# Attention probabilities kept 160 columns wide and turned in four row quarters

## The reference

```
B, H, S, D = 2, 8, 768, 64            # n_global 8, n_local 96
scores = q @ k.T / sqrt(D) + bias     # bias: -slope[h] * distance
keep = (pos_k < n_global) | ((rel >= 0) & (rel < n_local))
a = softmax(where(keep, scores, -1e9))
x = a @ v                             # (B, S, H * D) = (2, 768, 512)
h = relu(x @ w_in)                    # d_ff = 1024
x2 = (h * sigmoid(conv3(h))) @ w_out
g = relu(x2 @ w_in2);  u, v = halves of g
out = (u * (w_spatial @ layernorm(v) + b_spatial)) @ w_out2
```

## Time and profile before

| what | value |
|---|---|
| median of 3 runs (lowest, highest) | 361.33 us (361.33, 361.51) |
| the profiled execution | 361.26 us, span of its instructions 359.5 us |
| PE busy | 351.6 us, 2891 matmuls |
| DVE, ACT, POOL busy | 215.7, 177.7, 89.2 us |
| granted clock of PE, mean | 1.000 |

### The profile page before, as it was taken

How to read it: one execution, slowest core, us unless ns; L and a number is a source line. 1 busy time by engine, 2 the same in 40 slices (tenths; PEclk the granted TensorE clock), 3 DMA queues, 4 the chain that set the end, 5 groups by cost and what they waited for, 6 DMA issues and landing times.

```text
span 359.5 us, 7397 instructions
## 1 busy us (share of the span) xinstructions
PE 351.6 (98%) x2891; PEld 321.8 (90%) x2891; DVE 215.7 (60%) x572; ACT 177.7 (49%) x451; POOL 89.2 (25%) x165
## 2 busy tenths in 40 slices
PE   7889999999999999999999999999999999999996
PEld 3558989998899999999889999998999999998885
DVE  6896898778776697789693942115853444441000
ACT  4887668776767688652464622114652111112112
POOL 4899796445554000000120300003400000000000
PEclk9999999999999999999999999999999999999999
DMA  7962342333314033302000000010341000001222
GB/s 215 400 238 67 97 122 83 123 129 113 112 46 162 2 117 119 116 19 100 0 2 1 2 0 0 2 43 2 119 133 45 0 0 2 0 2 60 106 100 94
DMA packets 12233, 27.77 MB, mean 77 GB/s; under 512 B 1568, under 2 KB 4256, under 8 KB 12192
## 3 DMA queue, kind: packets, MB, share of 16 engines
q1 hardware_dynamic: 11904, 27.10, 22.3%
q10 hardware_dynamic: 288, 0.13, 0.2%
HBM read 24.08 MB, written 3.15 MB: 76 GB/s over the span
## 4 chain that ended last, share of the span: by engine, by line
PE 92%; DVE 4%; DMA 1%; issue 1%; POOL 1%; ACT 0%; DVEq 0%
PE bank L1587 20%; PE bank L1589 20%; PE bank L1588 20%; PE bank L1543 19%; PE bank L1522 5%; PE bank L1498 5%; PE bank L1450 3%; DVE p_sb L1072 2%; DMA counts<-in_n_keys 1%; DVE denom L1081 0%; DVE xT L1094 0%; POOL p_sb L635 0%; ACT p_sb L735 0%; DVE table L1051 0%; DVE pt_sb L1089 0%
## 5 line engine op out<-in xcount | busy, mean ns | idle before, releaser
L1543 PE MATMUL bank<-xT,w_hi 128*128 128x384 f32 x256 | 69.5, 344 | 0.0
L635 POOL TENSOR_SCALAR p_sb<-p_sb,denom 128x256 f32<-128x256 f32 (+1 forms) x96 | 47.1, 508 | 38.2 <-DVE denom L1083 38.2
L735 ACT ACTIVATE p_sb<-p_sb,row_min 128x256 f32<-128x256 f32 (+1 forms) x96 | 46.3, 486 | 17.7 <-DVE row_min L1072 17.6
L1543 PEld LDWEIGHTS bank<-xT,w_hi 128*128 128x128 f32 x256 | 45.8, 188 | 0.3 <-issue 0.2
L1543 PE MATMUL bank<-xT,w_lo 128*128 128x384 f32 x128 | 44.0, 344 | 0.0
L1109 DVE SCALAR_TENSOR_TENSOR c_sb<-h_sb,conv_sb,c_sb 128x382 f32<-128x382 f32 (+1 forms) x64 | 42.6, 666 | 2.3
L1587 PE MATMUL bank<-g_hi,w_hi 128*128 128x386 f32 (+1 forms) x128 | 43.3, 338 | 0.0
L1589 PE MATMUL bank<-g_hi,w_lo 128*128 128x386 f32 (+1 forms) x128 | 43.2, 337 | 0.0
L1588 PE MATMUL bank<-g_lo,w_hi 128*128 128x386 f32 (+1 forms) x128 | 43.1, 337 | 0.0
L1072 DVE CUSTOM_DVE_ANT_0 p_sb<-bank,table 128x256 f32<-128x256 f32 (+1 forms) x96 | 33.0, 397 | 8.1 <-PE bank L1450 7.9
L656 POOL TENSOR_SCALAR rstd<-mean_var 128x1 f32<-128x1 f32 x12 | 4.7, 392 | 129.2 <-DVE mean_var L1137 129.2
(11 more groups left out here) (96 smaller groups left out, 784.1 us busy)
## 6 DMA issues: line engine op xcount, KB each, us to landing
stage<-in_weights SPq DMA_DIRECT2D x17, 512.0 KB, 3.3
v_sb<-in_v SPq DMA_DIRECT2D x8, 390.0 KB, 3.9
k_sb<-in_k SPq DMA_DIRECT2D x8, 384.0 KB, 4.2
out_dram<-out_sb SPq DMA_DIRECT2D x11, 256.0 KB, 2.0
q_sb<-in_q SPq DMA_DIRECT2D x13, 192.0 KB, 2.5
v_sb<-in_v SPq DMA_DIRECT2D x6, 260.0 KB, 3.7
k_sb<-in_k SPq DMA_DIRECT2D x5, 256.0 KB, 4.0
stage_late<-in_weights SPq DMA_DIRECT2D x2, 512.0 KB, 11.4
```

The costliest lines, as they stand in the source:

```text
L635: nc.gpsimd.tensor_scalar(probs_h, probs_h, denom[:, u % SLOTS, h:h + 1], 1.0, ALU.mult, ALU.mult).then_inc(scaled, 1)
L735: nc.scalar.activation(p_sb[:, u % SLOTS, h, 0:n], p_sb[:, u % SLOTS, h, 0:n], ACT.Exp, bias=row_min[:, u % SLOTS, h:h + 1], scale=-1.0, a ...
L1543: last = nc.tensor.matmul(h_bank(j)[:, 0:C], w, x, start=r == 0, stop=r == F1_GROUP - 1)
```

## The change

**Layout.** A row of probabilities now holds only the 160 columns that its quarter of 32 rows needs (`NEAR`), with 96 columns of zeros on either side (`PAD`). All four quarters are biased with one table, `near_table`, which ACT copies together at the start from four pieces of the old table. DVE clears the right pads after the table is built, before the first bias; POOL clears the left ones.

**Turning.** A block of 128 keys is turned by four transposes, one for each quarter of 32 rows; each reads 128 columns of its own window in the padded row, and the four write into four banks (`quarters`). Three units lie beside each other in these four banks, and so does the output of attention (`xt_ps`, the last 128 columns of three of them). In triples 0 to 3 PE waits before each turn for the copy of the unit before; in later triples it turns three units in a row, and ACT copies after the third. Weighing starts when all three are copied. Before the next triple is turned, PE waits for `x_copied`.

**Output.** ACT first copies the output of attention raw to SBUF (`copy_x`, `x_raw`); `round_x` and `rest_of_x` then read it there.

**Order.** Scores run three triples ahead from triple 4 on (in triple 4 a second scoring stands in the middle of the first layer's matmuls), the 24 matmuls of the first layer come in one run, and ACT's and DVE's orders follow. The warm-up has 6 matmuls, 32 transposes, and 3 and 3 matmuls.

```diff
-WARM = (8, 3, 3, 3)
+WARM = (6, 8, 3, 3)
+PAD = P - PART
+AT_X = TG * P
-        p_sb = att("p_sb", [P, SLOTS, 2, 2 * P])
+        near_table = att("near_table", [P, NEAR])
+        p_sb = att("p_sb", [P, SLOTS, 2, PAD + NEAR + PAD])
+        x_raw = att("x_raw", [P, 2, C])
+        quarters = psum("quarters", [P, 4, 512])
         def score_cols(u, h):
             p, tt = divmod(u, TG)
-            bank = banks[(2, 5)[h] if tt == 2 else (6, 7)[h] if p == 1 else h]
-            at_col = tt % 2 * 2 * P
-            return bank[:, at_col:at_col + keys(u)]
+            bank = banks[(6 if u == 2 or p in (2, 4) else 0) + h]
+            return bank[:, tt * NEAR:tt * NEAR + near(u)]
-        xt_ps = banks[4]
+        xt_ps = quarters[:, 0:TG, AT_X:AT_X + P]
+        def turned_ps(u):
+            at_col = u % TG * P
+            return quarters[:, :, at_col:at_col + 2 * blocks_of(u) * PART].rearrange("p s (m q) -> p m s q", q=PART)
-        ALONE = TG * (HP + 1)
+        ALONE = TG * (HP + 2)
...
+            nc.gpsimd.memset(p_sb[:, :, :, 0:PAD], 0.0).then_inc(pads, 1)
...
             def copy_pt(u):
-                act.wait_ge(turned, u + 1)
+                act.wait_ge(turned, u + 1 if u < GU else TG * (u // TG + 1))
                 wait_if(act, weighed, u + 1 - PT_SLOTS)
-                n = keys(u)
-                nc.scalar.copy(pt_sb[:, u % PT_SLOTS, :, 0:n], pt_ps(u)[:, :, 0:n]).then_inc(pt_in, 1)
+                nc.scalar.copy(turned_sb(u), turned_ps(u)).then_inc(pt_in, 1)
+            def copy_x(p):
+                wait_if(act, x_lo, p - 1)
+                wait_apart(act, weighed, TG * (p + 1))
+                nc.scalar.activation(x_raw[:, p % 2, :].rearrange("p (t n) -> p t n", t=TG), xt_ps, ACT.Copy
+                                     ).then_inc(x_copied, 1)
             def round_x(p):
-                wait_apart(act, weighed, TG * (p + 1))
-                nc.scalar.activation(xT[:, g % 2, 0, hp, :], xt_ps[:, 0:C], ACT.Copy).then_inc(x_hi, 1)
+                wait_apart(act, x_copied, p + 1)
+                nc.scalar.activation(xT[:, g % 2, 0, hp, :], x_raw[:, p % 2, :], ACT.Copy).then_inc(x_hi, 1)
...
             for u in range(GU):
                 if u < TG and not turned_on_dve(u):
                     copy_pt(u)
                 soften(u + TG)
+                if u % TG == 0 and u > 0:
+                    copy_x(u // TG - 1)
                 if u >= TG and not turned_on_dve(u):
                     copy_pt(u)
                 if u % TG == 0 and u > 0:
                     round_x(u // TG - 1)
             for p in range(HP, ALL_TRIPLES):
                 u = TG * p
+                copy_x(p - 1)
+                round_x(p - 1)
+                if p == HP:
+                    for tt in range(TG):
+                        soften(u + TG + tt)
                 for tt in range(TG):
-                    if p + 1 < ALL_TRIPLES:
-                        soften(u + TG + tt)
-                    if tt == 2:
+                    copy_pt(u + tt)
+                    if tt == 1:
                         relu_h(2 * (p - F1_FIRST))
-                    copy_pt(u + tt)
-                    if tt == 0:
-                        round_x(p - 1)
+                    if p + 2 < ALL_TRIPLES:
+                        soften(u + 2 * TG + tt)
                 relu_h(2 * (p - F1_FIRST) + 1)
+            copy_x(ALL_TRIPLES - 1)
             round_x(ALL_TRIPLES - 1)
...
             build_table()
+            nc.vector.memset(p_sb[:, :, :, PAD + NEAR:], 0.0).then_inc(pads, 1)
...
-            invert_sums(ALONE - 1, 1)
+            for u in range(GU + 2, ALONE):
+                invert_sums(u, 1)
+                if u + 2 < ALONE:
+                    bias_scores(u + 2)
             for p in range(HP, ALL_TRIPLES + 1):
                 u = TG * p
-                for tt in range(TG):
-                    if p + 1 < ALL_TRIPLES:
-                        bias_scores(u + TG + tt)
-                rest_of_x(p - 1)
                 if p == HP:
+                    rest_of_x(p - 1)
                     path_tests()
+                if p + 2 < ALL_TRIPLES:
+                    for tt in range(TG):
+                        bias_scores(u + 2 * TG + tt)
+                if p > HP:
+                    rest_of_x(p - 1)
...
             def turn_probs(u):
-                if u > GU and u % TG:
+                if u == 1:
+                    pe.wait_ge(pads, 2)
+                if 0 < u < GU:
                     wait_pt(pe, u - 1)
+                if u > 0 and u % TG == 0:
+                    pe.wait_ge(x_copied, u // TG)
+                n = blocks_of(u)
                 for h in range(2):
                     pe.wait_ge(scaled, 2 * u + h + 1)
-                    for c in range(0, keys(u), P):
-                        last = nc.tensor.transpose(pt_ps(u)[:, h, c:c + P], p_sb[:, u % SLOTS, h, c:c + P], ident[:])
+                    for k in range(n):
+                        for i in range(4):
+                            rows = slice(i * PART, (i + 1) * PART)
+                            at_key = PAD + k * P - (0 if n == 1 else i * PART)
+                            at_col = u % TG * P + (h * n + k) * PART
+                            last = nc.tensor.transpose(quarters[:, i, at_col:at_col + PART],
+                                                       p_sb[rows, u % SLOTS, h, at_key:at_key + P], ident[rows, rows])
                 last.then_inc(turned, 1)
             def weigh(u):
                 if tt == 0:
-                    wait_if(pe, x_lo, pg)
+                    wait_pt(pe, u)
+                    wait_pt(pe, u + 1)
+                    wait_pt(pe, u + 2)
...
             for p in range(ALL_TRIPLES):
                 for tt in range(TG):
                     turn_probs(TG * p + tt)
-                    if p == 0 and tt == 0:
-                        warm(WARM[3])
-                    if p == 0 and tt == 1:
-                        third_scores(1)
-                    if p >= F1_FIRST:
-                        for _ in range(F1_STEP // TG):
-                            f1(f1_next)
-                            f1_next += 1
-                if p + 2 < ALL_TRIPLES:
-                    scores(p + 2)
+                    if p < HP and tt == 1:
+                        scores(p + 2)
+                if p >= F1_FIRST:
+                    for i in range(F1_STEP):
+                        if p == HP and i == F1_STEP // 2:
+                            scores(p + 2)
+                        f1(f1_next)
+                        f1_next += 1
                 for tt in range(TG):
                     weigh(TG * p + tt)
+                if HP <= p < ALL_TRIPLES - 3:
+                    scores(p + 3)
```

More of the change, by code:

```diff
@@ L298, in build_program @@
         tables = sem("tables")
+        near_in = sem("near_in")
+        pads = sem("pads")
         path_in = sem("path_in")
@@ L314, in build_program @@
         scaled = sem("scaled")
+        x_copied = sem("x_copied")
         x_hi = sem("x_hi")
@@ L409, in place, with near, blocks_of, probs_of @@
             return g, g // 2, hp, tt, TG * (g % 2) + tt
-        def keys(u):
-            return P if place(u)[4] == 0 else 2 * P
+        def near(u):
+            return P if place(u)[4] == 0 else NEAR
+        def blocks_of(u):
+            return 1 if place(u)[4] == 0 else 2
+        def probs_of(u, h):
+            return p_sb[:, u % SLOTS, h, PAD:PAD + near(u)]
+        def turned_ps(u):
+            at_col = u % TG * P
+            return quarters[:, :, at_col:at_col + 2 * blocks_of(u) * PART].rearrange("p s (m q) -> p m s q", q=PART)
+        def turned_sb(u):
+            return pt_sb[:, u % PT_SLOTS, :, 0:blocks_of(u) * P].rearrange("p h (k s q) -> p (h k) s q", q=PART, s=4)
         def turned_on_dve(u):
@@ L810, in _ @@
             nc.scalar.activation(spare[:], minus_half[:], ACT.Exp, bias=minus_half[:], scale=-1.0)
+            act.wait_ge(tables, COUNT_STEPS + 3)
+            for i in range(4):
+                rows, at_col = slice(i * PART, (i + 1) * PART), AT_LATER + i * PART
+                nc.scalar.copy(near_table[rows, :], table[rows, at_col:at_col + NEAR]).then_inc(near_in, 1)
             for u in range(TG):
@@ L1072, in bias_scores @@
                     nc.vector.tensor_tensor_reduce(
-                        out=p_sb[:, u % SLOTS, h, 0:n], in0=score_cols(u, h),
-                        in1=table[:, at_col:at_col + n],
+                        out=probs_of(u, h), in0=score_cols(u, h),
+                        in1=table[:, AT_T0:AT_T0 + P] if t == 0 else near_table[:],
                         scale=slope(2 * hp + h) * UNIT, scalar=FAR, op0=ALU.add, op1=ALU.min,
@@ L1441, in score @@
                 g, _, hp, tt, t = place(u)
-                near = slice(0, P) if t == 0 else slice(part * PART, part * PART + NEAR)
                 at_key = (0, 0, 2 * P)[t] if t < TG else tt * 2 * P
+                first = at_key if t == 0 else at_key + part * PART
```

(23 more changed lines are left out.)

85 lines of the change are left out of this document (33 added, 52 removed).

## The result

The changed kernel takes 378.64 us (median of four runs, 377.62 to 379.78) against 361.33: the ratio is 1.048, 95% interval 1.045 to 1.051, so it is slower by 17.3 us. The forecast was 366.0 with a range of 362.2 to 373.5: the direction was right, the time lies 5 us above the range. The profiled run took 378.83 us, its span is 377.0.

What follows compares the result with a forecast made beforehand. An engine loop paces the kernel up to 28.92 us, PE's own instructions afterwards. Terms 1.7 + 3.7 + 2.4 - 3.7 + 0.4 - 0.5 + 0.3 + 0.3 = +4.6 on 361.3 give 366.0 us, range 362.2 to 373.5.

Steps and rivals of the forecast that it cites:

- If it falls to 1.2 GHz: Triples 1 to 3: if waits drop PE's clock, weighing and turns take about 1.2 us more per triple; chance 0.11.
- D: Rival: PE's longer waits in the loop of triples 1 to 3 lower the granted clock, giving 369.6 us; chance 0.11.
- case E: Rival: only instruction issue limits the quads, 0.027 us each less, -3.3 us, giving 362.7 us; chance 0.06.
- Triples 1 to 3: Shared PSUM banks close a loop of turns, copies and weighing: 6.14 us a triple against 4.92, +3.7 us.
- Triple 4: Work queued on ACT and DVE delays x's split to T + 3.9 and the weighing to T + 9.2: +2.4 us.
- Start: DVE's clearing of right pads before its first bias, 1.2 us, plus 0.5 in the first triple: +1.7 us.
- nothing to hide it: Start: the pad clearing on DVE, 1.2 us, delays the first bias in full.
- Triples 5 to 15: PE's own instructions set the pace: -3.7 in triples 5 to 12, +0.2 each in 13 and 14, -0.5 in 15.
- a quad: Four turns of 32 rows with 32 moving columns, replacing one full turn; expected 0.054 us at 2.4 GHz.
- cover 0.15 us; I take nothing: Triples 5 to 15: the weighing's wait for ACT's third copy, 2.2 us, is hidden by 2.36 us of PE work.
- Case B: Rival: a quad costs 0.107 us even at full clock, as the skill's load rule says, giving 373 us; chance 0.20.
- Case C: Rival: the loop of triples 1 to 4 does not close, a triple takes 4.5 us, giving 358.7 us; chance 0.16.

Runs made afterwards that it cites:

- e14: Changed kernel with zero matmuls filling PE's waits in triples 0 to 4, and PE's instructions shifted by 64 small matmuls ahead of the warm-up: 369.90 us, 1.0245.
- e1: Changed kernel with long matmuls on zeros added into PE's waits of triples 0 to 4 to hold the clock: 375.74 us, 1.040.
- e3: Changed kernel with zero matmuls in PE's waits (two ahead of the weighing) and DVE's bias of unit u + 4 put first: 374.61 us, 1.035.
- e6: e3 plus ACT's copies ahead of its exps from triple 4, triple 4's low part of x earlier, right pads cleared on GpSimd: 368.94 us, 1.021.
- e5: e3 with 64 small matmuls ahead of the warm-up in place of four long ones, shifting PE's instructions: 368.76 us, 1.022.
- e9: Changed kernel with only the shift: 64 small matmuls ahead of the warm-up, four long warm-up matmuls taken out: 375.54 us, 1.036.
- e12: e11 with right pads cleared on GpSimd behind the near table and the three fillers ahead of the first turn dropped: 363.38 us, 1.0054.
- e7: Changed kernel with only the right pads cleared on GpSimd instead of DVE: 378.77 us, 1.048.
- e4: Changed kernel with ACT's three copies of turned units ahead of its exps from triple 4 on: 374.51 us, 1.037.
- e11: e6 with PE's instructions shifted, two units' exps moved to triple 5, pads cleared between GpSimd's query scalings, near table split between ACT and GpSimd: 363.82 us, 1.007.

## Why the prediction was wrong

- **The step that failed: "If it falls to 1.2 GHz" was a rival at 0.11, and its price was too low.** The forecast held the clock at 2.4 GHz through waits that it had itself worked out as half of each triple. D is what happened. It was priced at 1.2 us in each of three triples on top of 366; measured against e14, the loops lose 23.71 - 18.95 = 4.8 us, 1.6 in each triple, triple 4 0.9 and the start 2.8, and the last two hold a second cause, below.
- **A step that was not there: PE's supply of instructions.** The change makes four turns out of one, and the forecast priced them by pitch only; case E's "only issue limits" is another matter. The stand of 1.27 us at 14.50 and two short ones in triples 7 and 8 (0.7 us together, against e14) are in the changed kernel; e1, e3 and e6 met 2.9 to 3.5 us. That supply is the cause is shown by three things: the stands lie also where the program has no wait (e1), they end at a like distance behind a transfer, and the shift takes them away where it is the one edit (e3 against e5, e1 against e14, the changed kernel against e9). The Trainium skill, "Runtime: NRT & Kernel Launch", section "Instruction fetch mechanics", has the blocks of 256 instructions that the trace shows, and says that the fetch is mostly hidden; where this PE ran dense small matmuls it was not, by up to 3.5 us.
- **Triples 1 to 3: the mechanism was right.** The order of the chain came as written, and with clock and instructions supplied it takes 6.32 us on average (forecast 6.14), +4.2 instead of +3.7. The missing 0.5 is one link, from ACT's third copy to the weighing: 0.82, 0.82 and 0.71 us in the three triples instead of 0.61. The copy's 0.56 is in both; PE follows its end by 0.26 us (0.14 in triple 3), not by 0.05. ACT's copy and PE's weighing of triple 2 in e14:

```profile
25.98 0.56 ACT L760 COPY pt_sb<-quarters 128x512 f32<-128x512 f32 x1
...
26.80 1.31 PE L1560 MATMUL quarters<-pt_sb,v_sb 128*64 128x128 f32 x20 [0.28 <-ACT pt_sb L760]
```

- **Triple 4: right in kind, too small.** With both supplied, the weighing comes 10.1 us after the first turn, 3.3 later than before instead of 2.4; x is split 4.4 us after it instead of 3.9. (The stretch in the table has +4.3, with the second scoring.) That the order of ACT's and DVE's queues is the cause is shown by e6 and e12: with other orders the weighing comes 6.45 us after the turn; in the kernel before it was 6.81.
- **Start: +1.9 with both supplied, forecast +1.7.** That is close by luck in part. The clearing took 1.02 us (estimate 1.2), but "nothing to hide it" was wrong: e7 shows the near table beside it, done as late (7.63 us in the changed kernel, the clearing 7.56), so taking the clearing away gains nothing. The +1.9 also holds e14's stand of 0.35 us and its other warm-up.
- **Triples 5 to 15: a quad passes at 0.062 us at 2.4 GHz, forecast 0.054.** PE in triple 10 of the changed kernel, first turn, first and 24th first-layer matmul:

```profile
95.21 0.82 PE L1536 MATMUL quarters<-ident,p_sb 32*128 32x32 f32 x40
95.96 0.62 PE L1581 MATMUL bank<-xT,w_hi 128*128 128x384 f32 x2
...
100.05 0.34 PE L1581 MATMUL bank<-xT,w_lo 128*128 128x384 f32 x1
```

  By the starts in the trace, the second of these ten quads follows the first by 0.086 us and the others follow each other by 0.062 to 0.064; the change of tiling behind the last turn takes 0.15 (forecast 0.20). To the 24th matmul it is 4.84 us here (5.21 before, forecast 4.80) and 4.97 with twelve quads (forecast 4.87). That is 0.6 us less gain in triples 5 to 12. The wait for the low part of x in triples 8 and 12 takes 0.5 instead of 0.3. The rest of the missing 1.9 us (-1.5 in e14, forecast -3.4) is the step "cover 0.15 us; I take nothing": the weighing does wait for the third copy, 1.1 us over triples 5 to 12 in e14, and with the copies first (e4, e12) it doesn't.

  Case B is refuted. The Trainium skill, "TensorE: Matmul & The Clock Gate", section "LDWEIGHTS (loading the stationary operand)", prices one load of 128 columns at 0.107 us, with few rows as with many; with the four loads of a quad side by side, as the forecast took them, that would make 0.107 us a quad, an estimate. Here it is 0.062, and 0.107 is what quads take at half the clock, in the warm-up as in triple 4 of the changed kernel at a granted clock of 0.50; the measurement decides. Case E's 0.027 is refuted by the same starts.
- **Case C** (the loop doesn't close) is refuted: the changed kernel's loops take 7.8 to 8.1 us, 6.2 to 6.4 with clock and instructions supplied. Only with DVE's order mended too do they come to 5.36, still above the 4.92 of before and C's 4.5.

What stays open: why the stands end 1.2 to 1.6 us after the landing (one of 0.47 us in e11 and e12 ends 0.2 to 0.3 after it), why the fetch at 20.8 to 21.1 us starts only 0.6 to 1.1 us after PE has stopped in e1, e3 and e6 (the DMA engines are full there, but just as full in e5, where it came in time), and what in the start holds the first turn at 9.56 in e12. It is also open what about the loop lets the clock fall. The fillers both shorten PE's waits and give it long matmuls in place of small ones, and no run has the one without the other; that the clock costs what it costs is shown, that the waits alone bring it down is not.

## What to carry to other kernels

A change that saves work on a full engine but ties its stages into one chain is paid where that engine isn't full. There the loop also cost PE its clock: the fillers that held it were worth 5.6 us (e9 against e14). So such a loop has to be priced at half the clock as a likely case, not as a remote one. Count instructions as well as microseconds: four small matmuls for one use up four times the instruction supply, and a stand that the profile calls "issue", or gives to a releaser that was long done, is worth a test by shifting the program by some hundred instructions. In queues that several stages share, what another engine waits for goes ahead of what is needed a triple later.

## What was not expected of the hardware

A short step on DVE that starts beside one long GpSimd instruction can last until that ends. Timeline of the kernel after in triple 2, then of e11 at the start:

```profile
24.06 1.27 POOL L670 TENSOR_TENSOR w_lo<-stage,w_hi 128x512 fp32r<-128x512 f32 x1
24.09 1.26 DVE L1114 TENSOR_SCALAR denom<-denom 128x2 f32<-128x2 f32 x1 [0.30 <-ACT p_sb L752]
...
25.38 0.17 DVE L1116 RECIPROCAL denom<-denom 128x2 f32<-128x2 f32 x1
```

```profile
4.44 1.15 DVE L1092 TENSOR_SCALAR reach<-key,count_f 128x32 f32<-128x32 f32 x1
4.50 1.06 POOL L660 MEMSET p_sb<- 128x1152 f32 x1
```

Two columns of `denom` took 1.26 us here, to within 0.02 us of GpSimd's end. Of the 28 such steps of the kernel after, 22 take 0.16 to 0.20 us; the other six (0.30 to 1.26 us) each end within 0.04 us of a GpSimd instruction. The step at 4.44 takes 0.30 us in the kernel after and took 1.15. So in e11 the first bias came at 7.15 us, at 6.39 in e7, and the first turn at 10.40: a clearing put into a gap of GpSimd's queue was not free. The bias, which reads PSUM, kept its 0.29 us beside a clearing of the same size in e7.
